# A fused local attention and gated expert: 20 chunks of 832 tokens become one stream of 16 chunks of 1014 tokens and one of 419

## What is computed

```python
# 1: local attention, over the token and the six before it
w = softmax(weight_gen, axis=-1)                     # 4 x 4160 x 8 x 7
out = einsum('bshk,bskhg->bshg', w, x_unf)           # x_unf: 7 rows of x for each token
# 2: gated expert
h = maximum(out @ w_in, 0)                           # 192 -> 1024
conv_out[s] = sum_k conv_w[k] * h[s - 1 + k]         # three taps, zeros outside a batch
result = (h * sigmoid(conv_out)) @ w_out             # 1024 -> 192
```

## Time and profile before

| | |
|---|---|
| median of 3 runs | 767.01 us (765.59 to 767.22) |
| profiled execution, its own time | 767.54 us |
| its span (first to last instruction) | 765.8 us |
| granted clock of PE over the span | 0.98 of full |
| transfers | 43.50 MB, 57 GB/s |

### The profile page before, as it was taken

How to read it: one execution, slowest core, us unless ns; L and a number is a source line. 1 busy time by engine, 2 the same in 40 slices (tenths; PEclk the granted TensorE clock), 3 DMA queues, 4 the chain that set the end, 5 groups by cost and what they waited for, 6 DMA issues and landing times.

```text
span 765.8 us, 10644 instructions
## 1 busy us (share of the span) xinstructions
PE 707.7 (92%) x4021; PEld 681.8 (89%) x4021; DVE 666.6 (87%) x646; ACT 526.1 (69%) x723; POOL 610.6 (80%) x308
## 2 busy tenths in 40 slices
PE   1655899999999999999999999999999999999998
PEld 0444898999989999989999899999899998999998
DVE  6898899999999999999999999999999998986550
ACT  2257678676787767786767877677867677776761
POOL 4989979798999888897889998888978888962320
PEclk9788899999999999999999999999999999999999
DMA  9700131221403031313214030313132120000001
GB/s 207 184 0 1 35 85 31 71 67 42 106 16 84 16 91 44 85 28 74 71 37 106 16 86 16 90 44 85 26 75 70 37 75 28 21 16 26 13 27 37
DMA packets 28301, 43.50 MB, mean 57 GB/s; under 512 B 5507, under 2 KB 25594, under 8 KB 25852
## 3 DMA queue, kind: packets, MB, share of 16 engines
q1 hardware_dynamic: 28250, 42.82, 22.1%
HBM read 30.03 MB, written 12.78 MB: 56 GB/s over the span
## 4 chain that ended last, share of the span: by engine, by line
PE 78%; ACT 9%; POOL 5%; issue 4%; DVE 3%; DMA 1%; SPq 0%; DVEq 0%; POOLq 0%; ACTq 0%
PE out_ps L763 39%; PE z L749 33%; PE turn_ps L776 3%; ACT hidden L487 2%; POOL gated L295 2%; PE z L805 2%; POOL weighted L295 2%; ACT gated L505 1%; DVE attn L631 1%; ACT L505 1%; ACT L511 1%; ACT z L494 1%; DMA mask<-in_masks 1%; ACT expo L511 1%; POOL gated L445 1%
## 5 line engine op out<-in xcount | busy, mean ns | idle before, releaser
L295 POOL TENSOR_TENSOR weighted<-x_win,soft 120x1344 f32<-120x1344 f32 x133 | 365.3, 2752 | 75.8 <-DVE attn L631 75.6
L763 PE MATMUL out_ps<-wo,gated 128*128 128x192 f32 x2016 | 351.2, 328 | 8.1 <-issue 6.1
L763 PEld LDWEIGHTS out_ps<-wo,gated 128*128 128x128 f32 x2016 | 328.1, 188 | 14.4 <-issue 12.0
L487 ACT ACTIVATE hidden<-z 128x836 f32<-128x836 f32 x160 | 138.9, 868 | 167.6 <-PE z L749 141.0
L445 POOL TENSOR_TENSOR gated<-gated,hidden 128x832 f32<-128x832 f32 x119 | 197.6, 1666 | 46.2 <-ACT gated L505 46.1
L631 DVE TENSOR_REDUCE attn<-weighted 120x192 f32<-120x1344 f32 x133 | 205.3, 1545 | 0.0
L601 DVE SCALAR_TENSOR_TENSOR z<-hidden,cw,z 128x832 f32<-128x832 f32 x160 | 171.8, 1074 | 18.2 <-ACT z L494 16.9
L607 DVE SCALAR_TENSOR_TENSOR z<-hidden,cw,z 128x832 f32<-128x832 f32 x160 | 174.0, 1087 | 4.3
L494 ACT ACTIVATE z<-hidden,cw 128x832 f32<-128x832 f32 x160 | 153.4, 959 | 5.2
L749 PE MATMUL z<-xa_hi,wa_hi 128*128 128x418 f32 x320 | 108.8, 422 | 15.4 <-ACT gated L505 8.4
L505 ACT ACTIVATE gated<-z 128x832 f32<-128x832 f32 x119 | 101.9, 856 | 13.5 <-DVE z L607 12.7
(11 more groups left out here) (66 smaller groups left out, 430.6 us busy)
## 6 DMA issues: line engine op xcount, KB each, us to landing
x_win<-in_x SPq DMA_DIRECT2D x18, 1170.0 KB, 8.1
out<-out_sb SPq DMA_DIRECT2D x127, 96.0 KB, 1.6
logits<-in_weight_gen SPq DMA_DIRECT2D x18, 183.8 KB, 7.8
x_win<-in_x SPq DMA_DIRECT2D x1, 1160.2 KB
x_win<-in_x SPq DMA_DIRECT2D x1, 1092.0 KB
wo<-in_moe_w_out SPq DMA_DIRECT2D x1, 768.0 KB, 14.2
gated<-in_moe_w_in SPq DMA_DIRECT2D x1, 512.0 KB, 8.3
gated<-in_moe_w_in SPq DMA_DIRECT2D x2, 256.0 KB, 9.9
```

The costliest lines, as they stand in the source:

```text
L295: return engine.tensor_tensor(y, rows, s, ALU.mult)
L487: nc.scalar.activation(hidden[:, r, :].rearrange("p (a b) -> p a b", a=2), both(r, HALF), ACT.Relu).then_inc(s_hidden, 1)
L763: last = nc.tensor.matmul(out_ps[0:end - u * P, 0:D], gated[:, j, u * P:end], wo[:, j, :], start=(j == 0), stop=(j == J - 1))
```

## The change

The four batches become one stream, with one token that belongs to no batch between two batches (the masks make its attention zero, and it is not stored). The stream of 16643 tokens is divided into 16 chunks of 1014 tokens and a last one of 419. A full chunk lies on 127 partitions with eight tokens each, 1016 columns; the product into `z` is ten matrix products of 508 columns. The last chunk has four tokens per partition on 106 partitions, one PSUM bank, and five products of 424 columns.

- The rings of three chunks (`x_win`, `xa_hi`, `xa_lo`, `xb`, `mask`, `inverse`, `gated`) become rings of two; `z`, `hidden` and `weighted` stay at three. Since `gated` has two, ACT's sigmoid of a chunk's first step waits for the tiles of the chunk before the last.
- Each full chunk has exactly eight tiles (seven of 128 tokens and one of 118), one in each step. In the first tile of a chunk PE waits for each gated part by itself.
- Exponentials are taken for groups of 1, 2, 5, 5 and 4 chunks. The maxima and the subtractions of a group of five stand in five steps, one in each.
- `LEAD` is 12. Rounds of transposes stand at other slots and in part ahead of the product in their step (see `ROUNDS`: first and last token, part, then the slots of PE, ACT and DVE).
- Chunk 0: DVE does two of eight products. The load of x is cut so that its first eight rows land by themselves; the mask and the logits of chunk 1 are loaded ahead of x; the exponentials of chunks 1 and 2 are one instruction, ahead of the casts of `w_in` on ACT; ACT takes the parts of `w_in` ahead of the first round of transposes.
- A transfer whose partitions are no multiple of 16 is cut in two, and a transfer that crosses from one batch to the next in several.

```diff
-CHUNK = 832
-RING = 3
-GROUP = 7
-LEAD = 13
+SIZE = 1014
+TOKENS = 8
 AHEAD = 2
-SOFTMAX_SECOND = -9
-LOAD = -8
-LOAD_W = -10
-STALL = 0
-BY_VECTOR = 2
 OUTS = 4
+SLOTS = 8
+EARLY = 5
+ROUNDS_FIRST = [(0, 4, "a"), (0, 4, "b"), (4, 6, "ab"), (6, 8, "ab")]
 POOL_STEPS = (0, 1, 3, 4, 6, 7)
-SLOTS = 8
+BY_VECTOR = {0: (2, 4), 1: ()}
+OWN_BUFFERS = 5
+FIRST_ROWS = 8
+GROUPS = [(0,), (1, 2), (3, 4, 5, 6, 7), (8, 9, 10, 11, 12), (13, 14, 15, 16)]
+GROUP_SLOTS = 5
+STALLS = {}
+LEADS = {}
+LEAD = 12
+ROUNDS = [(0, 4, 'a', 4.5, 5.5, 5.5), (0, 4, 'b', 6.5, 7.5, 7.5), (4, 8, 'a', 8, 8.5, 8.5), (4, 8, 'b', 9, 9.5, 9.5)]
...
+class Chunk:
+
+    def __init__(self, number, begin, size, tokens, step):
+        self.number = number
+        self.begin = begin
+        self.size = size
+        self.tokens = tokens
+        self.parts = -(-(size + 2) // tokens)
+        self.cols = self.parts * tokens
+        self.banks = -(-self.cols // 512)
+        self.step = step
...
+    stream = batch * (seq + 1) - 1
+    found, begin, step = [], 0, 0
+    while begin < stream:
+        number, size = len(found), min(SIZE, stream - begin)
+        tokens = TOKENS if size + 2 > TOKENS // 2 * P else TOKENS // 2
+        step += STALLS.get(number, 0)
+        found.append(Chunk(number, begin, size, tokens, step))
+        begin += size
+        step += 8
+    return found
 
...
+        cut = p0 + (p1 - p0) // 16 * 16
+        return [(a, b) for a, b in ((p0, cut), (cut, p1)) if b > a]
...
+    TILE_STEP = {c.step + J + v: t for t, (c, v) in enumerate(TILES) if c is not LAST}
...
+        return c.step - LEADS.get(c.number, LEAD)
...
+    SUM_AT, TURN_AT, TAKE_AT, LOW_AT = {}, {}, {}, {}
+    for c in CHUNKS[1:]:
+        for i in range(c.tokens):
+            SUM_AT.setdefault(start_of(c) + i, []).append((c, i))
+        for r, (first, stop, kinds, *slots) in zip(range(len(c.rounds)), ROUNDS):
+            for table, slot in zip((TURN_AT, TAKE_AT, LOW_AT), slots):
+                table.setdefault(start_of(c) + slot, []).append((c, r))
...
+            def load_logits(c):
+                if group_of(c) in GROUPS[2:]:
+                    sp.wait_ge(s_exp, len([g for g in GROUPS if g[-1] < c.number]))
+                for a, b, offset, n, row in logit_pieces(c):
+                    if offset and a == 0 and c is FIRST:
+                        sp.wait_ge(s_cleared, 1)
+                    sp.dma_start(logits[a:b, slot_of(c), offset * HK:(offset + n) * HK],
+                                 bass.AP(w_flat.tensor, row * HK, [[c.tokens * HK, b - a], [1, n * HK]])) \
+                        .then_inc(s_logits[slot_of(c)], 16)
...
+            load_logits(FIRST)
+            load_mask(FIRST)
+            load_logits(CHUNKS[1])
+            load_x(FIRST)
+            for d in GROUPS[1][1:]:
+                load_logits(CHUNKS[d])
+            load_weights()
+            load_mask(CHUNKS[1])
+            load_x(CHUNKS[1])
             sp.dma_start(wo[:, :, :], w_out.rearrange("(j p) d -> p j d", p=P)).then_inc(s_weights_out, 16)
...
+            for k in range(FIRST_STEP, LAST_STEP + 1):
+                for c in CHUNKS[2:]:
+                    if group_of(c) in GROUPS[2:] and k == start_of(CHUNKS[group_of(c)[0]]) - 17:
+                        load_logits(c)
+                    if k == start_of(c) - 10:
+                        load_mask(c)
+                        load_x(c)
...
+                for c, i in SUM_AT.get(k + AHEAD, []):
+                    if i not in by_vector(c):
                         product(c, i)
...
+                    if i == TOKENS - 1 and c is not LAST:
+                        normalise_next(c)
+                for c in CHUNKS[2:]:
+                    f = CHUNKS[group_of(c)[0]]
+                    if group_of(c) in GROUPS[2:] and k == start_of(f) - 10 + slot_of(c):
+                        pool.wait_ge(s_top, c.number + 1)
+                        subtract_top(nc.gpsimd, c)
+                n = STEP_OF.get(k - 1)
+                if n is not None and on_pool(n):
+                    apply_gate(n)
+
+            for d in GROUPS[1][:1]:
+                pool.wait_ge(s_top, d + 1)
+                subtract_top(nc.gpsimd, CHUNKS[d])
+            for i in range(FIRST.tokens):
+                if i not in by_vector(FIRST):
+                    product(FIRST, i)
+                if i == 3:
+                    for d in GROUPS[1][1:]:
+                        pool.wait_ge(s_top, d + 1)
+                        subtract_top(nc.gpsimd, CHUNKS[d])
+            normalise_next(FIRST)
+            for k in range(FIRST_STEP, LAST_STEP + 1):
...
+                if n % J == 0 and c.number >= 2:
+
+                    act.wait_ge(s_out_ps, TILES_BEFORE[c.number - 1])
...
+                if g in GROUPS[2:]:
+                    act.wait_ge(s_soft, f.number)
...
+            exponent(GROUPS[0])
+            exponent(GROUPS[1])
             split_weights()
-            exponent(Chunk(0, 1), 1, slice(1, 2))
             take_conv_weights()
             act.wait_ge(s_conv_weights, 1)
-            take_turned(Chunk(0, 0), 0)
             take_rest()
-            for r in range(1, len(ROUNDS)):
-                take_turned(Chunk(0, 0), r)
-            pipeline(step)
-            for (turn, u), bank in zip(last_tiles(), last_banks()):
-                take_out(turn, u, bank)
+            for r in range(len(FIRST.rounds)):
+                take_turned(FIRST, r)
+            for k in range(FIRST_STEP, LAST_STEP + 1):
...
             def attention_first():
-                c, after = Chunk(0, 0), Chunk(0, 1)
-                softmax_begin(c)
+                c = FIRST
+                maxima(c)
+                dve.wait_ge(s_top, 1)
+                subtract_top(nc.vector, c)
+                maxima(CHUNKS[1])
                 sums(c)
-                reciprocals(c)
                 normalise(dve, nc.vector, c)
-                first_product(c, BY_VECTOR)
+                own_product(c, 2)
+                for d in GROUPS[1][1:]:
+                    maxima(CHUNKS[d])
+                own_product(c, 4)
                 sum_taps(c, 2)
                 sum_taps(c, 0)
-                softmax_begin(after)
                 sum_taps(c, 1)
                 sum_taps(c, 3)
-                sums(after)
-                reciprocals(after)
                 sum_taps(c, 4)
+                sums(CHUNKS[1])
                 low_part(c, 0)
+                low_part(c, 1)
                 sum_taps(c, 5)
-                low_part(c, 1)
                 sum_taps(c, 6)
+                sum_taps(c, 7)
                 low_part(c, 2)
                 low_part(c, 3)
 
...
+                width = c.cols // c.banks
                 for m, (weights, moving) in enumerate(parts):
-                    for half in range(2):
-                        last = nc.tensor.matmul(z[r][:, half, 0:HALF], weights,
-                                                moving[:, half * HALF:(half + 1) * HALF],
+                    for bank in range(c.banks):
+                        last = nc.tensor.matmul(z[n % 3][:, bank, 0:width], weights,
...
+            def out_parts(t, bank, steps):
+                c, v = TILES[t]
+                begin, end = c.ring * SIZE + v * P, c.ring * SIZE + min(v * P + P, c.size)
+                for j in steps:
+                    if v == 0 and c is not LAST:
+                        gated_ready(c.number * J + j)
+                    last = nc.tensor.matmul(bank[0:end - begin, 0:D], gated[:, j, begin:end], wo[:, j, :],
+                                            start=(j == 0), stop=(j == J - 1))
+                return last
...
+                n = STEP_OF.get(k + 2)
+                for c, r in TURN_AT.get(k, []):
+                    turn(c, r)
+                if n is not None:
+                    product_in(n)
+                for c, r in TURN_AT.get(k + 0.5, []):
+                    turn(c, r)
+                if k in TILE_STEP:
+                    product_out(TILE_STEP[k])
```

More of the change, by code:

```diff
@@ new lines, in shifted, with gated_flat, gated_banks, columns @@
+        def shifted(c, n, tap):
+            return hidden[:, n % 3, tap:tap + c.size].rearrange("p (a b) -> p a b", a=c.banks)
+        def gated_flat(c, n):
+            return gated[:, n % J, c.ring * SIZE:c.ring * SIZE + c.size]
+        def gated_banks(c, n):
+            return gated_flat(c, n).rearrange("p (a b) -> p a b", a=c.banks)
+        def columns(buffer, c, part):
+            return buffer[:, c.ring, 0:c.cols].rearrange("p (a i) -> p a i", i=c.tokens)[:, :, part]
+        def turned(c, r, q):
+            part, kinds = c.rounds[r]
+            cols = (part.stop - part.start) * c.parts
+            return bank_of(c, r)[:, q * cols:(q + 1) * cols].rearrange("p (i a) -> p a i", a=c.parts)
@@ L328, in local_attention_gated_expert, with logits_landed @@
+        def logits_landed(c):
+            return 16 * sum(len(logit_pieces(d)) for d in CHUNKS if d.number <= c.number and slot_of(d) == slot_of(c))
```

889 lines of the change are left out of this document (406 added, 483 removed).

## The result

The changed kernel takes **754.08 us** (median of 4 runs, 752.75 to 755.22), beside 767.12 (765.59 to 767.54) for the kernel before on the same chip: a ratio of 0.9833, 95% interval 0.981 to 0.9856. The forecast was 745, with a range of 736 to 759: the sign and the range hold, and 9 us are missing. The profiled run took 752.75, its span is 751.0 (765.8 before).

The account below looks back on a forecast made before the run. PE was taken as the bound: first tile done at 91.5 us, then 645.6 of PE work to 737.1, with 2.4 behind and 4 of waits a span of 743.5, so a time of 745 us. The range was 736 to 759.

Parts of the forecast that it names:

- Product into `z`: PE's ten merged instructions per product: 2.32 us, ends 2.31 and 2.35; 0.98 us in the last chunk.
- Transposes: PE's transposes in the steps: 0.113 us each, scaled by 127/120; 228 after the first tile, 25.8 us.
- The other engines keep up: Steady chunks: DVE 38.1 us, POOL 36, ACT at most 4.0 a step; PE's step of 5.14 stays the bound.
- the idle 2.5 us of a ring: PE's idle time at the end of each three-chunk ring, in steps without a tile, would lose its cause.
- Waits: Small waits together: 4 us allowed, ends 0 and 16; longer exponentials hidden, or about 1 us each without cover.
- Start: Up to the first tile's end: POOL begins at 9.7 us, first product near 39, tile done at 91.5 (89 to 94.5).
- Rival 2: In the start, the casts' delay reaches POOL or maxima and subtractions add up: 5 to 10 us, 753; chance 0.09.
- End: After the first tile PE's work runs to 737.1 us; 2.4 follow, and the last chunk's short steps leave room.
- The sum: Whole kernel: PE's work to 737.1 us, with 2.4 behind and 4 of waits, gives a span of 743.5.
- 1 (the idle stays): In the rings a wait replaces the steps without tiles; all 15.8 us of PE's idle time return: 757; chance 0.22.
- 3: Round 4's transposes wait for DVE's low part: 2.2 us a chunk, 31 us over 14 chunks, 774; chance 0.06.
- 4: PE is not the step's bound; DVE's step is 5.1 to 5.2 us: 748 to 755; chance 0.05.

Follow-up runs that it names:

- e2: Changed kernel with DVE doing one product of chunk 0 in place of two, POOL seven: 751.96 us, ratio 0.9817.
- e12: Changed kernel with DVE doing none of chunk 0's eight products, POOL all eight: 752.04 us, ratio 0.9816.
- e4: Changed kernel with the last eight tiles alternating between two PSUM banks: 752.01 us, ratio 0.9814.

## Why the prediction was right in sign and 9 us short

Point by point, by its own steps.

**Product into `z`: right, and better than taken.** I took 2.32 us between 2.31 and 2.35; it is 2.30. The 19 ns above the columns are a cost per instruction: 418 columns took 193 ns, 508 take 230, and 508 / 2.4 GHz is 212, so 18 ns come on top. That is 2.3 us below the forecast over 117 products. The rule of the Trainium skill ("TensorE: Matmul & The Clock Gate", "Wait — 56ns, not 53.3ns?") gave 214 ns; the trace disagrees by 16 ns an instruction, on which most of the gain of merging them rests.

**Transposes: mis-sized by a little.** I took 0.107 us for 120 columns from the difference of two steps, 0.32 us for three, and scaled it to 0.113. The scaling was right (0.103 and 0.108 us from start to start), the base was not: three transposes put off the tile behind them by a little more than their own time. By the difference of two steps again, 5.33 and 4.91, it is 0.42 us for four, 0.105 each; the balance takes 0.107, which is 1.4 us less in 228.

**The other engines keep up: right, but not by the margin that the sums showed.** DVE's 38.1, POOL's 36 and ACT's at most 32 us a chunk are 37.8, 36.1 and 28.8 in the 41 us of the steady window. But these are sums of busy time, and the run with seven tiles shows that what the others need is a loop through all of them, 40.8 us a chunk in this order, 0.1 below PE's 40.94. The forecast that the idle 2.5 us of a ring go was right: there are steps without tiles no more, and with one put back PE idles again. By the same run, though, a further cut of PE's work in one step of a steady chunk would have bought next to nothing, which "93% of PE's step, as before" did not say. An even cut in all eight steps was not tried.

**Waits: the total was right by luck, the reason for it wrong.** I allowed 4 us, and the stalls of the middle are 3.9. But I had called the longer exponentials "hidden, since a `z` bank has over a step to spare". The buffer with nothing to spare was another: the one PSUM bank of the tiles, which each step now fills, and whose copy stands behind the sigmoid and the exponentials on ACT. What I gave as the price without cover, 1 us each, was 2.15 and 1.5. The run with the copy first shows that it was this bank: 0.45 us is left of the two stalls. For an instruction that gets longer, every buffer that the instructions behind it release had to be looked at, not only the one its own step frees.

**Start: the step that failed.** POOL at 9.7 (measured 9.86) was right. "POOL's work covers it: its fourth product of chunk 1 needs only DVE's first sum" was wrong: POOL's first product of chunk 1 already needs sum 5 of chunk 0, since `weighted` has three buffers, and DVE gave that sum only behind its low part, which waited for ACT's casts. The run with the casts first gives 3.3 us of it, near the middle of "up to 6 us if that cover is gone". The casts themselves were later than forecast, 23.52 for 21, because DVE's two products held POOL's up (the next point), and the first product was at 41.56, not 39. For the end of the first tile I had 91.5; it is at 95.85. Of these 4.35 us 3.05 are there at the end of the first gating (60.65 for 57.6). From there on the sum was about right, though it stopped at the eighth gating and called that the tile: in the kernel before, the eighth gating ends at 85.79 and the tile 4.5 us later (it took 4.2 us itself, at a granted clock of 0.60), in the changed kernel at 95.25 and only 0.6 later, since PE begins it ahead of the last part, at the full clock. Then PE is idle 3.7 us more before the second tile, which I had not counted. Together that is 8.1 us. Rival 2 named this place and 753 us, and I gave it 0.09.

**DVE's own product.** The 46.0 us that I carried over from before held one product of DVE's beside POOL's; I counted nothing for what the second does to POOL, and the pair e2 and e12 show 2.28 us for one. A sign stood in the rows: POOL's six products from 11.02 are 2.95 us each, where the group's mean is 2.75.

**End: mis-sized.** I gave it nothing but the 2.4 us behind the last copy. It has some 3.2 us more, of which 2.1 are tiles in one bank without a product between them, as the two banks show. The rest was not followed.

**The sum.** 743.5 for the span, + 8.1 for the start, - 3.7 for products and transposes, - 0.1 for the waits, + 3.2 at the end: 751.0. What was left out at the end and what was taken too dear for PE nearly cancel, which is luck too: that is why the start alone seems to make up the 9 us.

**The rivals.** 1 (the idle stays) is there by two thirds of its amount, 10.8 of 15.8 us, but in the start, behind exponentials and at the end, not in each ring. 2 is the one that came. 3 did not: PE doesn't wait for a hand-off of transposes in the steady part. 4 did not come, though the run with seven tiles shows how near it was: 0.1 us a chunk.

## What to carry to other kernels

Before a cut in the busiest engine's work is counted, ask what the loop through the other engines and their buffers allows: leave one piece of that work out and see whether the time falls. A piece taken out of one step and a little taken out of each are two questions. An engine can't use a step in which it alone has less to do, so even out the steps first. When an instruction on a shared engine becomes longer or is moved ahead of others, go through every buffer that the instructions behind it release, and look for the one that has a single copy.

## What was not expected of the hardware

- Elementwise products on DVE and POOL hold each other up nearly one for one, and the one that begins second is held up. POOL's two products took 7.33 us beside one of DVE's and 5.05 alone (e2, e12). In the changed kernel DVE's first began at 12.25 and took 2.56 us, POOL's second began at 12.31 and took 4.83; in e4 POOL's began first, at 12.32, and took 2.59, and DVE's began at 12.45 and took 4.75. The sums of DVE didn't show this: the fourth product of POOL in e12 ran beside one and the begin of another (17.26 and 18.73) and took 2.61 us.
- A matrix product of these operands costs 18 to 19 ns above its columns at the full clock, with 418 columns as with 508, and at 1.2 GHz nothing that the rows show.
- A tile of 118 tokens takes PE as long as one of 128, 2.60 us.
- Leaving out 2.60 us of PE's 40.94 in a chunk shortened the chunk by 0.1 us.
